# First tile's q in rows of 64 a head with zeros, asked for by ScalarE, and one more filler matmul

## The reference

```python
# q, k, v, alpha: (4, 8, 768, 48) float32
state = zeros((B, H, D, D))
for t in range(S):
    state = alpha[:, :, t, :, None] * state + einsum('bhd,bhe->bhde', k[:, :, t], v[:, :, t])
    y[:, :, t] = einsum('bhd,bhde->bhe', q[:, :, t], state)
x = y.transpose(0, 2, 1, 3).reshape(B * S, H * D)      # 3072 x 384
h = x @ w_in1;  x = (h - tanh(h)) @ w_out1             # 384 -> 2048 -> 384
h = x @ w_in2;  out = (max(h, 0) + alpha2 * min(h, 0)) @ w_out2
```

## Time and profile before

| | us |
|---|---|
| median of 3 runs | 929.26 |
| lowest and highest | 928.76, 930.33 |
| the profiled execution | 929.27 |
| its span | 927.6 |
| TensorE busy | 906.6 (98%) |
| VectorE busy | 564.7 (61%) |
| ScalarE busy | 327.2 (35%) |
| GpSimd busy | 210.3 (23%) |

### The profile page before, as it was taken

The page is one execution under the profiler, slowest core; times in us unless marked ns, Lnnn a source line. Parts: engine busy times, 40 slices in busy tenths (PEclk is TensorE's granted clock), DMA queues, the critical chain, the costliest instruction groups (busy, mean ns, idle before and its releaser), DMA issues.

```text
span 927.6 us, 22784 instructions
## 1 busy us (share of the span) xinstructions
PE 906.6 (98%) x9915; PEld 744.8 (80%) x9915; DVE 564.7 (61%) x724; ACT 327.2 (35%) x536; POOL 210.3 (23%) x193
## 2 busy tenths in 40 slices
PE   5799999999999999999999999999999999999998
PEld 4688788888888888878888888888888888888886
DVE  7898848656774776487344454565555555555553
ACT  6853634354344425433444521211211211212211
POOL 7654504332350434044214420000000000000000
PEclk9999999999999999999999999999999999999999
DMA  8532072034205312420072020100100100100000
GB/s 281 149 139 96 2 218 81 3 78 140 82 3 136 114 50 59 160 81 2 2 265 76 1 69 0 34 34 0 68 0 0 68 0 0 68 0 0 35 1 34
DMA packets 24965, 61.05 MB, mean 66 GB/s; under 512 B 3216, under 2 KB 11408, under 8 KB 22352
## 3 DMA queue, kind: packets, MB, share of 16 engines
q1 hardware_dynamic: 24672, 59.07, 20.5%
q10 hardware_dynamic: 208, 0.72, 0.3%
HBM read 46.15 MB, written 9.44 MB: 60 GB/s over the span
## 4 chain that ended last, share of the span: by engine, by line
PE 96%; issue 1%; DMA 1%; POOL 1%; ACT 1%; DVE 0%; POOLq 0%; DVEq 0%
PE ph L797 43%; PE acc L806 14%; PE acc L807 14%; PE acc L808 14%; PE ps L567 4%; PE ps L650 1%; DMA q_early<-q 1%; PE ps L561 1%; PE ps L554 1%; PE py L650 1%; POOL k_t L1351 1%; PE ph L650 1%; PE py L729 0%; PE ps L729 0%; PE ph L643 0%
## 5 line engine op out<-in xcount | busy, mean ns | idle before, releaser
L1012 ACT ACTIVATE g_hi<-g 128x512 fp32r<-128x512 f32 x192 | 121.2, 631 | 423.9 <-PE acc L808 335.8
L1271 DVE TENSOR_TENSOR g_lo<-g,g_hi 128x512 fp32r<-128x512 f32 x192 | 142.1, 740 | 193.7 <-ACT g_hi L1012 193.0
L806 PE MATMUL acc<-g_lo,w_hi 128*128 128x512 f32 x576 | 226.5, 393 | 0.0
L807 PE MATMUL acc<-g_hi,w_lo 128*128 128x512 f32 x576 | 224.3, 389 | 0.0
L808 PE MATMUL acc<-g_hi,w_hi 128*128 128x512 f32 x576 | 224.2, 389 | 0.0
L797 PE MATMUL ph<-x_hi,w_lo 128*128 128x512 f32 x573 | 164.4, 395 | 0.5 <-DVE w_lo L1246 0.5
L797 PE MATMUL ph<-x_hi,w_hi 128*128 128x512 f32 x576 | 162.1, 390 | 0.0
L797 PE MATMUL ph<-x_lo,w_hi 128*128 128x512 f32 x576 | 161.9, 389 | 0.0
L806 PEld LDWEIGHTS acc<-g_lo,w_hi 128*128 128x128 f32 x576 | 108.1, 188 | 23.7 <-DVE g_lo L1271 0.6
L797 PEld LDWEIGHTS ph<-x_hi,w_hi 128*128 128x128 f32 x576 | 108.0, 188 | 22.9
L808 PEld LDWEIGHTS acc<-g_hi,w_hi 128*128 128x128 f32 x576 | 108.1, 188 | 22.8
(11 more groups left out here) (156 smaller groups left out, 626.5 us busy)
## 6 DMA issues: line engine op xcount, KB each, us to landing
v_t<-v SPq DMA_DIRECT2D x6, 1024.0 KB, 6.3
a_t<-alpha SPq DMA_DIRECT2D x5, 1024.0 KB, 7.0
k_t<-k SPq DMA_DIRECT2D x5, 1024.0 KB, 5.2
x<-x_out SPq DMA_DIRECT2D x6, 768.0 KB, 8.0
x_in<-x SPq DMA_DIRECT2D x6, 768.0 KB, 4.9
kT<-trees SPq DMA_DIRECT2D x64, 64.0 KB, 2.0
q_w<-q SPq DMA_DIRECT2D x10, 384.0 KB, 5.7
out<-prob SPq DMA_DIRECT2D x5, 768.0 KB, 3.8
```

What stands on the lines that cost most here:

```text
L806: pe.matmul(acc[:, m, :], w_hi[:, f, part], g_lo[:, f % 2, :], start=(f == 0), stop=False)
L807: pe.matmul(acc[:, m, :], w_lo[:, f, part], g_hi[:, f % 2, :], start=False, stop=False)
L1012: act.activation(g_hi[:, f % 2, :], g[:, f % 2, :], ACT.Copy).then_inc(g_hi_made, 1)
L1271: dve.tensor_tensor(g_lo[:, f % 2, :], g[:, f % 2, :], g_hi[:, f % 2, :].bitcast(F32), ALU.subtract).then_inc(g_lo_made, 1)
```

## The change

- The host makes one more array, `q_tile0`: the first tile's q in 64 rows a head, the last 16 of them zeros. A q transfer of the first tile is now 64 rows of 4 KB, and brings the zeros with it.
- What is cleared of each place is only the half of the partitions that no transfer writes. No transfer waits for a clearing.
- SP asks for alpha and k of each lane and goes on to the first weights. ScalarE asks for both pieces of lane 0's q at its start, and for those of lane 1 between the third and the fourth copy of lane 0's factors.
- VectorE's `start_lane` waits for three of the four factors.
- GpSimd's tree product of lane 0 stands one mask select earlier.
- A third filler matmul ("busy", 7, 1) stands at the end of the list's entry for level 7, after lane 1's level 6 and ahead of the first Y; it writes `py` and has no waits of its own.

```diff
--- before.py
+++ after.py
@@ -88,6 +88,7 @@
            [("Y", 1, 0), ("Y", 1, 1)]]
 
 BEFORE[LEVELS - 1].insert(0, ("busy", 6, 2))
+BEFORE[LEVELS - 1].append(("busy", 7, 1))
 
 BEFORE[LEVELS + 2].append(("half", 0, 0))
 BEFORE[1].append(("clear", 0, 0))
@@ -177,7 +178,7 @@
         eng.wait_ge(sem, value)
 
 
-def attention_mlp(nc, q, q_first, a_odd, k, v, alpha, w_in1, w_out1, w_in2, w_out2, alpha2, x1, out):
+def attention_mlp(nc, q, q_tile0, q_first, a_odd, k, v, alpha, w_in1, w_out1, w_in2, w_out2, alpha2, x1, out):
     with ExitStack() as ctx:
         def sb(name, shape, dt=F32):
             return ctx.enter_context(nc.sbuf_tensor(name, shape, dt))
@@ -422,13 +423,7 @@
                 xs = xs_of(lane)
                 cols = slice(xs.start * C, xs.stop * C)
                 sp.dma_start(a_t[:, cols], alpha[0:128, cols]).then_inc(ld_a[lane], 16)
-
-                if lane == 1:
-                    sp.dma_start(k_t[:, cols], k[0:128, cols]).then_inc(ld_k[lane], 16)
-                for hh in range(lane + 1):
-                    sp.wait_ge(zeroed, 1 if lane == 0 else hh + 2)
-                    sp.dma_start(q_early[64 * hh:64 * hh + D, xs, hh, :],
-                                 q[hh * D:hh * D + D, cols].rearrange("p (x t) -> p x t", x=XL)).then_inc(ld_q[lane], 16)
+                sp.dma_start(k_t[:, cols], k[0:128, cols]).then_inc(ld_k[lane], 16)
 
             def load_v(a):
 
@@ -732,13 +727,15 @@
                                            start=True, stop=True)
                 mm.then_inc(st_done, 1)
 
-            def busy(count):
-
-
-                pe.wait_ge(w_hi_made, 1)
-                pe.wait_ge(masked[1], 5)
+            def busy(e, count):
+
+
+                to = acc[:, 1, :] if e == 6 else py[:, :]
+                if e == 6:
+                    pe.wait_ge(w_hi_made, 1)
+                    pe.wait_ge(masked[1], 5)
                 for _ in range(count):
-                    pe.matmul(acc[:, 1, :], w_hi[:, 0, 0:128], w_hi[:, 0, 0:512], start=True, stop=True)
+                    pe.matmul(to, w_hi[:, 0, 0:128], w_hi[:, 0, 0:512], start=True, stop=True)
 
             def first_term(f, cols):
 
@@ -753,7 +750,7 @@
                     if what == "Y":
                         first_y(lane, l)
                     if what == "busy":
-                        busy(l)
+                        busy(lane, l)
                     if what == "half":
                         pe.wait_ge(w_lo_made, 1)
                         pe.wait_ge(x_hi_made, DUO)
@@ -831,6 +828,14 @@
                 act.activation(q_w[rows, xs_of(lane), 1 - hh, :], zeros_over([XL, C], rows), ACT.Copy).then_inc(
                     pads_cleared[lane], 1)
 
+            def load_q(lane, hh):
+
+                xs = xs_of(lane)
+                rows = slice(64 * hh, 64 * hh + 64)
+                act.dma_start(q_early[rows, xs, hh, :],
+                              q_tile0[rows, xs.start * C:xs.stop * C].rearrange("p (x t) -> p x t", x=XL)
+                              ).then_inc(ld_q[lane], 16)
+
             def clear_prob(lane):
 
                 heads = slice(DUO * H * lane, DUO * H * (lane + 1))
@@ -843,7 +848,7 @@
 
                 act.activation(left_totals(lane, l), halves_of(lane, l)[0], ACT.Copy).then_inc(left_copied[set_of(lane)], 1)
 
-            def copy_first_factors(lane, product):
+            def copy_first_factors(lane, product, steps=range(2)):
 
                 tree = tree_of(lane, 1 if product else 0)
                 if product:
@@ -853,7 +858,7 @@
                 else:
                     act.wait_ge(ld_a[lane], 16)
                     frm, to = (in_fours(tree)[:, :, 2], in_fours(tree)[:, :, 1]), (0, 1)
-                for step in range(2):
+                for step in steps:
                     act.activation(first_factors(lane, step)[:, :, to[step]], frm[step], ACT.Copy).then_inc(left_copied[lane], 1)
 
             def copy_plain(lane):
@@ -1021,14 +1026,15 @@
 
             act.sem_inc(acc_read, KT)
             act.sem_inc(stored, 16)
-            first = slice(0, XL * C)
-            act.dma_start(k_t[:, first], k[0:128, first]).then_inc(ld_k[0], 16)
+            for hh in range(2):
+                load_q(0, hh)
             act.wait_ge(zeroed_pool, 1)
-            act.dma_start(q_early[64:64 + D, xs_of(0), 1, :],
-                          q[D:2 * D, first].rearrange("p (x t) -> p x t", x=XL)).then_inc(ld_q[0], 16)
             clear_pads(0, 0)
-            copy_first_factors(0, False)
-            copy_first_factors(0, True)
+            copy_first_factors(0, False, range(2))
+            copy_first_factors(0, True, range(1))
+            for hh in range(2):
+                load_q(1, hh)
+            copy_first_factors(0, True, range(1, 2))
             passes(act, layer, first_tile, attention, split, weights)
 
         @block.vector
@@ -1057,7 +1063,7 @@
             def start_lane(lane):
 
                 dve.wait_ge(ld_q[lane], 32)
-                dve.wait_ge(left_copied[lane], LANE_FACTORS)
+                dve.wait_ge(left_copied[lane], 3)
                 begin_lane(lane, 0)
 
             def begin(step):
@@ -1285,11 +1291,11 @@
                 attention([w for w in work if w[0].endswith("_late")], a)
 
 
-            dve.memset(q_heads[:, 0, xs_of(0), :], 0.0).then_inc(zeroed, 1)
+            dve.memset(q_heads[64:128, 0, xs_of(0), :], 0.0).then_inc(zeroed, 1)
             dve.memset(g[:, 0, 0:DM], 0.0).then_inc(g_cleared, 1)
             clear_pads(0, 1)
             for hh in range(2):
-                dve.memset(q_heads[:, hh, xs_of(1), :], 0.0).then_inc(zeroed, 1)
+                dve.memset(q_heads[64 - 64 * hh:128 - 64 * hh, hh, xs_of(1), :], 0.0).then_inc(zeroed, 1)
             clear_pads(1, 0)
             dve.sem_inc(g_made, 2)
             dve.sem_inc(g_lo_made, 2)
@@ -1434,7 +1440,7 @@
                 pool.tensor_tensor(w_lo[:, f, :], raw(which, f), w_hi[:, f, :].bitcast(F32),
                                    ALU.subtract).then_inc(w_lo_made if which else w_lo_pool, 1)
 
-            pool.memset(q_heads[:, 1, xs_of(0), :], 0.0).then_inc(zeroed_pool, 1)
+            pool.memset(q_heads[0:64, 1, xs_of(0), :], 0.0).then_inc(zeroed_pool, 1)
             pool.memset(ident[:, :], 0.0)
             pool.memset(masks, 1.0)
             pool.drain().then_inc(const, 1)
@@ -1449,7 +1455,7 @@
             pool.drain().then_inc(const, 1)
             pool.wait_ge(const, 2)
             for l in range(1, LEVELS - 1):
-                if l == 3:
+                if l == 2:
                     pool.wait_ge(ld_a[0], 16)
                     product(0, 1)
                 half, nb = half_and_blocks(l)
@@ -1512,6 +1518,7 @@
 
     arrays = {
         "q": np.ascontiguousarray(ordered(rows(q))),
+        "q_tile0": np.ascontiguousarray(ordered(padded(q)[0:128])),
         "q_first": np.ascontiguousarray(padded(q).reshape(TILES * 128, -1, 4)[:, :, ORDER[0:2]].reshape(TILES * 128, -1)),
         "a_odd": np.ascontiguousarray(padded(alpha)[:, 1::2]),
         "k": padded(k),
```

## The result

| | before | after |
|---|---|---|
| median of 21 runs each, in turn | 928.95 | 930.62 |
| lowest and highest | 927.35, 930.88 | 929.79, 932.03 |
| the profiled execution | 929.27 | 930.32 |
| its span | 927.6 | 928.6 |

The ratio is 1.0018, with a 95% interval from 1.0012 to 1.0025. The kernel became slower by 1.67 us. That is just inside the 1.86 us called "no change" ahead of the result, but the interval lies wholly above 1, and the time is outside the predicted range of 925.8 to 929.2.

What follows compares the result with a forecast made beforehand. TensorE, busy 98% of the span, was taken as the bound, with gains possible only before 44 us. 929.27 less 1.25 (head) less 1.3 (clock rise by the filler) gave 926.7 us, range 925.8 to 929.2.

Steps and rivals of the forecast that it cites:

- Where the time is decided: Whole kernel: TensorE is solid after 44 us, so each microsecond won or lost before that counts whole.
- By 4.5 us 0.86 MB is in: Loading at the head: bytes moved by then, at 382 GB/s from 2.25 us, towards lane 0's 1.57 MB.
- I take 7.1 for its last byte: Loading at the head: lane 0 complete between 6.2 and 7.6 us, taken as 7.1.
- about 7.2: Head: start of TensorE's first scores, instead of 8.47, a gain of 1.25 us.
- Who keeps up: Head: factors, VectorE's first product and ScalarE's copy would be ready for the earlier q, with half a microsecond of cover.
- Lane 1's q "between 11.3 and 13.7": Lane 1's loading: landing time, taken as 12.5 us, covered because it is needed by 14.05.
- The filler: Gap before the first Y: the matmul of 0.58 us fits, and an earlier clock rise wins 1.3 us, 1.6 at most.
- B: Rival on the head, chance 0.12: transfers give nothing, lane 0 complete only at 8.3 or lane 1's q past 14; 929.2 us.
- at 8.4 nothing is gained: Head: the ceiling of harm, the latest start of TensorE's first scores that the prediction allowed for.
- C: Rival on the Ys, chance 0.12: the clock rises later against the work, making the kernel slower, 931.4 us.

Runs made afterwards that it cites:

- e8: Changed kernel with `q_tile0` given as the last input instead of the second, no instruction differing; median 929.11 us, ratio 1.0005.
- e14: Changed kernel, new array last, SP asking for lane 1's alpha and k and the weights only once lane 0's q is in; 928.67 us, ratio 1.0.
- e9: Kernel before with the new array as second input, only a small read of it at the very end; 930.14 us, ratio 1.0015.
- e12: Kernel before with the new array as last input, only a small read of it at the very end; 928.69 us, ratio 0.9999.
- e6: Kernel before, its waits, queues and clearings kept, with q's pieces of 64 rows read from the new array; 930.92 us, ratio 1.0023.
- e5: Kernel before with q's pieces of 48 rows read from the new array; 929.62 us, ratio 1.0012.
- e2: Changed kernel, SP asking for lane 1's alpha and k and the weights only once lane 0's q is in; 930.24 us, ratio 1.0012.
- e1: Changed kernel with the queues and order of the kernel before, but 64-row pieces and no waits; 929.89 us, ratio 1.0004.
- e10: Kernel before, unchanged, run again as a measure of scatter; 928.30 us, ratio 0.9999.
- e3: Changed kernel without the third filler matmul; 931.00 us, ratio 1.0016.
- e16: Kernel before with the third filler matmul alone, repeated in another set; 927.46 us, ratio 0.9994.
- e4: Kernel before with the third filler matmul alone; 927.84 us, ratio 0.9986.

## Why the prediction was wrong

**Where the time is decided: right for this pair.** What stands after 44 us stayed as it was within its scatter, VectorE's dense stretch moved as a block, and lane 1's q was not critical. The loss at the head went through whole to the Ys (8.47 to 10.70 is 2.23, the first Y went from 38.00 to 40.21).

**The failed step: "By 4.5 us 0.86 MB is in", and the sum from it to "I take 7.1 for its last byte" and a start at "about 7.2".** The scores started at 10.70, 3.5 us later. The sum was wrong in two ways.

First, it took the 382 GB/s of the earlier trace rows as a rate that the edit would leave alone, and it was 260. With 1.57 MB to move, 0.06 in by 2.25 us and 255 to 260 GB/s, the bytes would all be in at 8.1 instead of 7.1.

Second, and larger, it counted every byte that the core moves as lane 0's, and put the time from the last byte to the start at 0.1. In after the core had moved 2.2 MB when lane 0's q was in, at 10.58. The kernel before could have shown this: it had moved lane 0's 1.44 MB in total by 7.1 us, and its q was in at 8.36, with 1.86 MB moved.

The runs give the parts, each from one profile: 1.75 us for the place of the array (10.70 to e8's 8.95), 0.75 for sharing the engines with lane 1 and the weights (8.95 to e14's 8.20), and the last 1.0, from 8.20 to 7.2, is nearly all the 0.95 us between the last bytes and the start in e14. There, with lane 0 alone and the array last, the bytes were in by 7.25, near the 7.1 forecast. The explanations tested, with their size:

- PLACE, 0.7 to 1.75 us at the head, 1.2 to 1.5 in the ratios: shown by two pairs without a differing instruction (after and e8, e9 and e12). The text took a new input to be free and named no rival for it. That a shift in memory is what does it is inferred from the order of the inputs, and why it slows them is open: no run records addresses, and three good and two bad placings make no rule.
- ROWS, 0.8 us at the head: e6 against e5, one profile each, at the bad place only; about what the additional bytes take at the rate of the time. The prediction drew from the Trainium skill, page "SBUF — State Buffer", section "Door 1: The DMA port swizzle", by which a 48-row piece already loads its fullest port with eight rows, that the zeros would be free. This measurement is against that conclusion: 250 GB/s with 64 rows and 245 with 48, so the zeros took time as any bytes do. Nor does e6 bear out that before's 209 GB/s from 4.5 to 7.5 us showed the half reach: with 64-row pieces in the same places it moves 272 there.
- CROWD, 0.44 us at the bad place (e2, with lane 1's q still sharing) and 0.75 at the good one (e14 against e8), paid back by lane 1's wait for k.
- ORDER gained nothing: 10.75 (e1) against 10.70. That earlier asking brings earlier landing did not come true: e6, with q's pieces asked for 0.4 and 0.8 us later than in e1, has its scores no later (10.41 against 10.75). The likely reason is that the moving limits q, not the asking. Here the Trainium skill's page "DMA: Bandwidth & Descriptors", section "Issuing engines are not separate DMA queues", which says that another issuer saves only the issuing, agrees with e1 and after. In the ratios the old order is even better (1.0004 against 1.0018, the intervals just meet), so a small loss by the new one isn't excluded.

At the good place and with the filler the change's early asking reaches 929.11 (e8, ratio 1.0005) where before with the filler has 927.84 and 927.46 (0.9986 and 0.9994): without the misplaced array it would still be no gain.

**Who keeps up: right and idle.** GpSimd's tree product came at 5.48 (before 5.86), the masks ended at 7.7, all four factors were in PSUM by 8.1. They wait for q 2.5 us more.

**Lane 1's q "between 11.3 and 13.7": not tested closely.** Its scores start at 15.53 behind lane 0's group, with no wait, so it was covered, as said; but the cover came from lane 0's own delay.

**The filler: right in kind, too large.** It fits the gap and brings the clock's rise ahead of the first Y. In the eleven profiles with it the 32 matmuls of the first Y take 1.08 to 1.11 us in ten and 1.36 in one (e1). Of the seven without it three are at 1.93 or 1.94 (before, e10, e12) and four at 1.08 (e3, e5, e6, e9). The three are those with an early head, at or under 8.82; the four have it at 9.51 or later. So behind a late head the early rise came without a filler: in the changed kernel, whose head is late, the filler won nothing that the runs show (e3), and with an early head it wins 0.9 to 1.2 in the medians (e16, e4). Why a late head helps is open; seven profiles show that they go together, no run sets them apart. Besides, the second Y doesn't gain its full share: the timeline of after has 0.37 us of idle inside it at 43.93, for which the profile names no releaser. From the first Y to the last x_hi it is 5.51 (after) and 5.50 (e4) against 6.11 and 6.19 (before, e10): 0.6 to 0.7 instead of 1.3.

**The rivals.** B, the transfers give nothing, named the right suspect and a far too small price: it took before's 8.3 as the worst for q, "at 8.4 nothing is gained", though an estimate of a transfer that nobody had seen can't be bounded by one that was changed. C foresaw a slower kernel by a later clock, and the clock came earlier. Slower came true, for a cause that no rival had. The range ended at 929.2 for that reason.

## What to carry to other kernels

- A new input may change every load of the others. Time it alone: the array added and not read, and added last. Put new inputs behind the old ones.
- A transfer rate read from a trace belongs to that set of pieces and that order of inputs. When an edit changes either, the ceiling of harm is not "as late as before".
- Asking earlier helps only if asking was late. Look whether the DMA engines are already full when the waited-for pieces are under way, and count what else is moved by the time they are in. Work the sum on the kernel before first: if it gives 7.1 where the trace has 8.36, a term is missing.
- A cheap matmul in the last gap before high-rate work made the rise of the clock dependable here; count its gain only where the rise would otherwise come late, and look at more than one profile for that.

## What the runs showed of the hardware that was not expected

- The same loads move 314 GB/s or 234, and 302 or 261, from 2 to 6 us, by the order of the inputs alone, with the DMA engines at 92 to 96% in all four.
- Pieces of 64 rows of 4 KB in half of the partitions move at the rate of those of 48 (250 and 245 GB/s), so that 16 rows of zeros a piece cost 0.8 us at the head.
- With lane 0 alone on the DMA engines, 0.95 us pass between the last of its bytes (by 7.25) and the matmul that waits for them (8.20).
- Without the filler the clock rises ahead of the first Y in the four profiles with a late head and some 3 us later in the three with an early one; with one matmul of 0.5 us in the gap it was ahead in ten of eleven.
